# When a gated tile's copy may start, and who makes the last T sums

## What is computed

```python
x = attn_out.transpose(0, 2, 1, 3).reshape(B * S, H * D)   # 1536 x 512
for e in range(4):
    h = np.maximum(x @ w1[e], 0.0)
    out += p[:, e:e + 1] * (h @ w2[e])
h = out @ w_in
g = h * (1.0 / (1.0 + np.exp(-1.702 * h)))
return g @ w_out
```

## Time and profile before

| | |
|---|---|
| runs | 826.63, 828.28, 823.92 us (median 826.63) |
| profiled execution | 824.39 us, of which the span 822.2 us |
| TensorE clock granted | 0.998 of full speed over the span, 9 tenths or more in each of 40 slices |
| PE, DVE, ACT, POOL busy | 97%, 69%, 52%, 71% of the span |
| DMA | 148.92 MB, mean 181 GB/s |

### The profile page before, as it was taken

How to read it: one execution, slowest core, us unless ns; L and a number is a source line. 1 busy time by engine, 2 the same in 40 slices (tenths; PEclk the granted TensorE clock), 3 DMA queues, 4 the chain that set the end, 5 groups by cost and what they waited for, 6 DMA issues and landing times.

```text
span 822.2 us, 14168 instructions
## 1 busy us (share of the span) xinstructions
PE 798.7 (97%) x4894; PEld 779.6 (95%) x4894; DVE 568.6 (69%) x1194; ACT 427.8 (52%) x943; POOL 580.8 (71%) x406
## 2 busy tenths in 40 slices
PE   5889999999999999999999999999999999999997
PEld 4778999999999999999999999999999999999997
DVE  5888656666665566687877877665666665677777
ACT  3865445445445454546545544434456553656663
POOL 3697765655666699678778685777488873588794
PEclk9999999999999999999999999999999999999999
DMA  9959547375444354446245343343544445373412
GB/s 265 285 122 338 214 196 235 141 262 216 159 179 175 141 214 161 171 155 232 104 184 198 122 198 142 142 189 143 217 160 187 175 172 205 104 293 143 165 66 77
DMA packets 39957, 148.92 MB, mean 181 GB/s; under 512 B 16208, under 2 KB 17360, under 8 KB 36688
## 3 DMA queue, kind: packets, MB, share of 16 engines
q1 hardware_dynamic: 39888, 148.03, 49.9%
HBM read 100.81 MB, written 47.21 MB: 180 GB/s over the span
## 4 chain that ended last, share of the span: by engine, by line
PE 76%; POOL 10%; issue 5%; ACT 4%; DVE 3%; DMA 1%; SPq 0%; ACTq 0%; DVEq 0%; POOLq 0%
PE bank L1651 25%; PE bank L1653 24%; PE bank L1652 24%; POOL wd_lo L809 2%; POOL h_raw L832 2%; POOL t_raw L832 2%; PE bank L1606 2%; ACT prob L949 1%; PE bank L1617 1%; PE bank L1643 1%; DMA v_cols<-v_t 1%; ACT xb_first_hi L1050 1%; POOL wu_lo L730 1%; POOL wd_lo L742 1%; ACT xb_last_hi L1074 0%
## 5 line engine op out<-in xcount | busy, mean ns | idle before, releaser
L1358 DVE TENSOR_TENSOR xa<-bank,xa 128x384 f32<-128x384 f32 x208 | 115.8, 556 | 136.7 <-PE bank L1653 133.9
L1651 PE MATMUL bank<-h_hi,wd_hi 128*128 128x384 f32 x448 | 150.5, 336 | 0.3 <-DVE xa L1356 0.2
L1653 PE MATMUL bank<-h_lo,wd_hi 128*128 128x384 f32 x448 | 149.8, 334 | 0.0
L1652 PE MATMUL bank<-h_hi,wd_lo 128*128 128x384 f32 x448 | 149.7, 334 | 0.0
L1040 ACT ACTIVATE h_hi<-bank 128x384 fp32r<-128x384 f32 x112 | 55.1, 492 | 136.9 <-DVE bank L1415 113.5
L742 POOL TENSOR_TENSOR wd_lo<-stage,wd_hi 128x1024 fp32r<-128x1024 f32 x27 | 65.2, 2413 | 82.9 <-ACT wd_hi L997 82.8
L809 POOL TENSOR_TENSOR wd_lo<-stage,wd_hi 128x512 fp32r<-128x512 f32 x60 | 85.9, 1437 | 40.2 <-ACT wd_hi L1087 39.5
L1651 PE MATMUL bank<-xb_other_hi,wu_hi 128*128 128x384 f32 x336 | 113.0, 336 | 0.8 <-ACT snap L1024 0.2
L1653 PE MATMUL bank<-xb_other_lo,wu_hi 128*128 128x384 f32 x336 | 112.3, 334 | 0.0
L1652 PE MATMUL bank<-xb_other_hi,wu_lo 128*128 128x384 f32 x336 | 112.3, 334 | 0.0
L1024 ACT ACTIVATE snap<-bank 128x384 f32<-128x384 f32 x141 | 69.2, 491 | 64.0 <-PE bank L1653 63.1
(11 more groups left out here) (120 smaller groups left out, 2078.7 us busy)
## 6 DMA issues: line engine op xcount, KB each, us to landing
stage<-weights SPq DMA_DIRECT2D x25, 1024.0 KB, 4.9
split<-wu_hi SPq DMA_DIRECT2D x24, 896.0 KB, 3.6
split<-wu_lo SPq DMA_DIRECT2D x24, 896.0 KB, 5.6
wu_hi<-split SPq DMA_DIRECT2D x23, 896.0 KB, 6.3
wu_lo<-split SPq DMA_DIRECT2D x23, 896.0 KB, 8.0
stage<-weights SPq DMA_DIRECT2D x23, 512.0 KB, 4.5
k_win<-k_w SPq DMA_DIRECT2D x8, 720.0 KB, 8.1
v_win<-v_w SPq DMA_DIRECT2D x8, 576.0 KB, 9.3
```

The source lines that it names most:

```text
L1358: nc.vector.tensor_tensor(at, y_bank(g, t), at, ALU.add).then_inc(y_taken, 1)
L1651: nc.tensor.matmul(dst, w_h, a_h, start=first, stop=False, skip_group_check=True)
L1652: nc.tensor.matmul(dst, w_l, a_h, start=False, stop=False, skip_group_check=True)
L1653: return nc.tensor.matmul(dst, w_h, a_l, start=False, stop=last, skip_group_check=True)
```

## The change

It has two parts.

**Behind pairs.** In the first step of a pair, the raw copy of C11 and C21 (column 0 of row 0) waits for T sum 1 of the pair before (`4 * q - 3`) and no longer for all four and for the low tiles. In the second step, C11 and C21 wait for the low part of T sum 4 alone, C22 and C12 for T sum 3. Also, in the last layer (g >= 32), DVE takes P2,0 before the low part of C12 and no longer behind it.

**The tail.** T sums 2 and 3 of the last pair are made by DVE, in two halves each, straight from the gated tile's bank (`sum_last`), and the raw copies of C22 and C12 of step 47 go. POOL makes T sum 4 and its low part. The takes of the last pair have an order of their own, `TAKES_LAST`: P1,1 goes far back, P6,0 ahead of P3,1, and P2 behind P7. PE's order stays.

```diff
+TAKES_LAST = (("P1", 0), ("P5", 0), ("P5", 1), ("P1", 1), ("P3", 0), ("P6", 0), ("P3", 1), ("P6", 1),
+              ("P7", 0), ("P7", 1), ("P2", 0), ("P2", 1), ("P4", 0), ("P4", 1))
...
         def taken(g0, name, d):
 
-            return takes(g0) + TAKES.index((name, d)) + 1
+            return takes(g0) + (TAKES_LAST if g0 == STEPS - 2 else TAKES).index((name, d)) + 1
...
-                    pool.wait_ge(tsum_done, at + 2)
+                    if g + 2 == STEPS:
+                        pool.wait_ge(tlast_done, 3)
+                        pool.wait_ge(raw_done, copied(g + 1, "C21"))
+                    else:
+                        pool.wait_ge(tsum_done, at + 2)
...
-            for n in (2, 3, 4):
-                sum_hidden(STEPS - 2, n)
+
+            sum_hidden(STEPS - 2, 4)
+            pool.wait_ge(thi_done, 4 * pair_of(STEPS - 2) + 4)
+            pool.wait_ge(tlo_done, 4 * pair_of(STEPS - 2) + 3)
+            hi, lo = moved_2(5)
+            nc.gpsimd.tensor_tensor(lo, hidden_sum(4), hi.bitcast(F32), ALU.subtract).then_inc(tlo_done, 1)
...
                 act.wait_ge(gated_done, ready(g, c))
+                if g + 1 == STEPS and c[2] == "2":
+
+                    act.wait_ge(tlast_done, {"C22": 2, "C12": 3}[c])
...
-                if c[2] == "1":
-                    wait_count(act, blo_done if g % 2 == 0 else tlo_done, len(TILES_2) * q if g % 2 == 0 else 4 * q)
-                    wait_count(act, tsum_done, 4 * q)
+                if c[2] == "1" and g % 2 == 0:
+                    wait_count(act, tsum_done, 4 * q - 3)
                 elif g % 2 == 0:
                     wait_count(act, tlo_done, 4 * q - 1)
-                else:
-                    wait_count(act, tsum_done, 4 * q)
+                elif c[2] == "1":
+                    wait_count(act, tlo_done, 4 * q)
+                else:
+                    wait_count(act, tsum_done, 4 * q - 1)
...
-                act.wait_ge(tsum_done, 4 * pair_of(g) + n)
+                if g + 2 == STEPS and n in (2, 3):
+                    act.wait_ge(tlast_done, n + 1)
+                elif g + 2 == STEPS and n == 4:
+                    act.wait_ge(tsum_done, 4 * pair_of(g) + 2)
+                else:
+                    act.wait_ge(tsum_done, 4 * pair_of(g) + n)
...
-                    copy_tile(g, "C22")
+                    if g + 1 < STEPS:
+                        copy_tile(g, "C22")
...
-                    copy_tile(g, "C12")
+                    if g + 1 < STEPS:
+                        copy_tile(g, "C12")
...
+            def sum_last(n, c):
+
+                f = int(c[1]) - 1
+                dve.wait_ge(gated_done, ready(STEPS - 1, c))
+                b = hidden_sum(1) if n == 2 else hidden_block(0, 1)
+                nc.vector.tensor_tensor(hidden_sum(n)[:, f, :], hidden(STEPS - 1, c), b[:, f, :], ALU.subtract
+                                        ).then_inc(tlast_done, 1)
...
                     take_product(g - 2, "P5", 1)
-                    low_tile(g - 1, "C12")
+                    if g < FFN0:
+                        low_tile(g - 1, "C12")
                     take_product(g - 2, "P2", 0)
+                    if g >= FFN0:
+                        low_tile(g - 1, "C12")
```

More of the change, by code:

```diff
@@ L262, in attention_moe_ffn @@
         tlo_done = sem("tlo_done")
+        tlast_done = sem("tlast_done")
         y_done = sem("y_done")
@@ L366, in takes, with summed @@
             return sum((len(TAKES) - IN_PAIR if x % 2 else IN_PAIR) if paired(x) else 8 for x in range(g))
+        def summed(g0, name, d):
+            return takes(g0) + TAKES.index((name, d)) + 1
         def taken(g0, name, d):
-            return takes(g0) + TAKES.index((name, d)) + 1
+            return takes(g0) + (TAKES_LAST if g0 == STEPS - 2 else TAKES).index((name, d)) + 1
         def plain(g):
@@ L417, in copied @@
         def copied(g, c):
+            if g + 1 == STEPS:
+                return 4 * (2 * pair_of(g) + 1) + {"C11": 1, "C21": 2}[c]
             return 4 * (2 * pair_of(g) + g % 2) + READY[c]
@@ L672, in _ @@
                         sp.dma_start(out[d, :, 0:SEQ], xa[0][:, d, :]).then_inc(out_done, 16)
-            for name, d in TAKES[IN_PAIR:]:
-                if name != "P3":
+            for name, d in TAKES_LAST:
+                if name in ("P2", "P6", "P7", "P4"):
                     i, c, first = ADDED[name]
@@ L1045, in high_tile @@
                 act.wait_ge(gated_done, ready(g, c))
+                if g + 1 == STEPS and c[2] == "2":
+                    act.wait_ge(tlast_done, {"C22": 2, "C12": 3}[c])
                 if paired(g0 - 1):
-                    act.wait_ge(y_done, taken(g0 - 2, {(0, "1"): "P1", (1, "1"): "P2", (1, "2"): "P3"}[g % 2, c[2]], 1))
+                    act.wait_ge(y_done, summed(g0 - 2, {(0, "1"): "P1", (1, "1"): "P2", (1, "2"): "P3"}[g % 2, c[2]], 1))
                 else:
@@ L1067, in high_sum @@
             def high_sum(g, n):
-                act.wait_ge(tsum_done, 4 * pair_of(g) + n)
+                if g + 2 == STEPS and n in (2, 3):
[4 more added lines that the diff above has]
+                    act.wait_ge(tsum_done, 4 * pair_of(g) + n)
                 if paired(g - 1):
-                    act.wait_ge(y_done, taken(g - 2, ("P5", "P6", "P7", "P4")[n - 1], 1))
+                    act.wait_ge(y_done, summed(g - 2, ("P5", "P6", "P7", "P4")[n - 1], 1))
                 else:
@@ L1083, in high_held @@
                 if paired(g - 1):
-                    act.wait_ge(y_done, taken(g - 2, name, 1))
+                    act.wait_ge(y_done, summed(g - 2, name, 1))
                 else:
@@ L1360, in take_product @@
             def take_product(g, name, d):
-                dve.wait_ge(y_done, taken(g, name, d))
+                dve.wait_ge(y_done, summed(g, name, d))
                 if name == "P6":
@@ L1495, in _ @@
                     gate(g, "C22")
[L1496 to L1502, removed]
-                        take_product(g - 1, "P5", 0)
+                    if g + 1 < STEPS:
+                        take_product(g - 1, "P5", 0)
+                        gate(g, "C21")
+                        add_c12(g)
+                        low_tile(g, "C21")
+                        gate(g, "C12")
+                        low_tile(g, "C22")
                     continue
@@ L1573, in _ @@
                     key_maxima(u)
+            sum_last(3, "C22")
+            gate(STEPS - 1, "C21")
+            add_c12(STEPS - 1)
+            sum_last(2, "C22")
+            low_tile(STEPS - 1, "C21")
+            gate(STEPS - 1, "C12")
+            sum_last(2, "C12")
+            take_product(STEPS - 2, "P5", 0)
+            low_tile(STEPS - 1, "C22")
+            low_tile(STEPS - 1, "C12")
             take_product(STEPS - 2, "P5", 1)
-            low_tile(STEPS - 1, "C12")
-            take_product(STEPS - 2, "P2", 0)
-            take_product(STEPS - 2, "P2", 1)
+            sum_last(3, "C12")
             low_sum(STEPS - 2, 2)
-            take_product(STEPS - 2, "P3", 0)
-            take_product(STEPS - 2, "P3", 1)
+            take_product(STEPS - 2, "P1", 1)
             low_sum(STEPS - 2, 3)
[L1582 to L1585, removed]
+            for name, d in TAKES_LAST[4:]:
                 take_product(STEPS - 2, name, d)
```

## The result

| | before | changed |
|---|---|---|
| median of 20 runs | 824.96 us (823.30 to 829.14) | 820.60 us (818.61 to 825.24) |
| ratio | | 0.9946, 95% interval 0.9935 to 0.9957 |
| span of the profiled execution | 822.2 us | 818.8 us |
| granted clock, mean | 0.998 | 0.992 |

The kernel is 4.5 us faster (0.54%; the interval is 3.5 to 5.4 us). Forecast were 5.9 us and a time of 820.7. The time hit, the gain is 1.4 us smaller; the median of the three runs that the forecast was taken from, 826.63, was 1.7 above that of 20 runs, which hid the miss.

The account below looks back on a forecast made before the run. PE, busy for 97% of the span, was taken as the bound, with gains only at its stops: 3.2 + 1.0 + 1.7 = 5.9 us off a 826.63 us median, forecast 820.7 (own range 818.5 to 822.5; eight in ten 817.0 to 824.3).

Parts of the forecast that it names:

- What bounds the kernel: Whole kernel: PE is busy 97% of the span, so gains come only where PE stands still or does less.
- Part one: Behind expert pairs: C11's earlier copy removes the stops at P7 and P7,0, 5 x 0.65 = 3.2 us.
- the room that I gave P7,0: Expert pairs: P3,1 and P6,0 taken by 391.5, where P7,0 wants that at 392.55; 1.0 us of room.
- Part two: Last layer, steps 42, 44, 46: P2,0 taken ahead of C12's low part removes P2,1's stop, 1.0 us.
- The list of what would be wrong: Signs: PE still waiting at P7, tail two-tile low part over 1.5 us, new stop at P3,0 or next pair's P1,0.
- Part three: Tail: P3,0 0.3 us late, P6,0 and P7,0 without waits, P4,1 1.8 earlier; 1.7 us in all.
- The rule on the shared port: Tail: two-SBUF-input DVE and SBUF-reading POOL instructions block each other; sums from banks cost 0.56 us whatever POOL does.
- A: Rival, tail: DVE's low parts meet POOL or a take sits between; 821.7 to 822.4 us, chance 0.12.
- B: Rival, expert pairs: one stop stays, 822.3 us; both stay, 823.9 us; chance 0.12.
- C: Rival: removed waits weren't the last ones and the tail's new sums cost their saving; 826.6 us, chance 0.03.
- D: Rival, tail: sums from banks as slow as 1.94 us, kernel slower, 829.4 us if part one gives nothing; chance 0.03.
- faster: Whole kernel: a gain past about 0.5%, here 4.1 us, that a measurement can tell from no change; chance 0.74.

Follow-up runs that it names:

- e1: Kernel before with only the new waits of the raw copies (`copy_tile`): ratio 0.9954 (0.9935 to 0.9972).
- e2: Kernel before with only P2,0 taken ahead of C12's low part in the last layer: ratio 0.9994 (0.9979 to 1.001).
- e4: Changed kernel without taking P2,0 ahead of C12's low part in the last layer: ratio to before 0.9933 (0.9908 to 0.9958).
- e9: Changed kernel with one more DVE instruction behind the tail's first sum: 0.47 us more up to P4,1.
- e10: Kernel before with `keep(g, 1)` ahead of C11's raw copy behind the expert pairs: steps 16 to 28 take 176.06 us, before 175.98.
- e5: Changed kernel with P4,0 taken ahead of C12's gate in the last layer: step 40 to the tail's P2,0 115.57 us, changed kernel 116.36.
- e3: Kernel before with only the tail's part of the change: ratio 0.9985 (0.9967 to 1.0003).
- e6: Changed kernel, POOL's weight sums of pairs 42, 44, 46 on 8 of 256 columns, rest left out: step 40 to P2,0 115.33 us, changed kernel 116.36.
- e7: Like e5, with `keep(g, 1)` ahead of P6's weights on ACT in step 47: ratio to before 0.9918 (0.9893 to 0.9943).
- e11: Like e7, with T sum 3's halves behind C22's and C12's low parts, P3,0's take ahead of T sum 3's low part: ratio to before 0.9925.

## Why the prediction was right, and where not

**What bounds the kernel.** Right: PE's stops were the whole of it, and every gain is one of them gone. Not right is that each stop is worth its length: that at P2,1 was worth nothing.

**Part one.** Right in place, path and size. Predicted were `keep` done 0.5 us before PE wants it (it is 0.6) and 3.2 us in all (3.16 in the changed kernel, 3.25 alone). One link came out better than I had it: T sum 3's low part, taken at 1.94 us as in the earlier trace rows, took 0.95, because it now begins 0.06 us before POOL's next sum and not into it (389.19 and 389.25 above); POOL's sum took 2.04 instead of 1.28. It is so in all five of these steps (0.95, and 2.02 to 2.04). So the room that I gave P7,0 was too small by a microsecond.

**Part two.** The step that failed is the term "0.26 us of stall and about 0.07 of slow start go, three times: 1.0 us". The mechanism at P2,1 was right (its step is 1.04 now), but I asked only what is due directly behind the swap (C11's adding, P5), and not what is late one step on. The low part of T sum 4 was in the trace before, at 1.16 us, beside a weight sum of POOL (761.02, above); P4,0's take ended 0.15 us before P1,0 of the pair began, and where PE waited for a take 0.14 to 0.15 passed from its end to the product's start (750.59 to 750.73, 764.39 to 764.54): no room at all. The list of what would be wrong named a stop "at P1,0 of the next pair", but no chance or term stood behind it. The measured term is 0.0, and e1, e2 and e4 show it from both sides; what came in its place is the new stop at P1,0, 0.25 and 0.29 us, and that at P7 of step 47, 0.21.

**Part three.** 1.67 us from P2,0 to P4,1, against 1.8 forecast (0.3 lost ahead of P3,0 and 2.1 gained from there; measured from there, 9.54 - 7.63 = 1.9). P6,0 and P7,0 have lost their waits, the sums from banks take 0.56 us, the low parts of T sums 2 and 3 0.94. The loss is there, nearly 0.3 in all as forecast, but only 0.16 of it is at P3,0; 0.05 and 0.07 are at P2,0 and P2,1, which I had taken for on time. That room was as narrow as P1,0's, and e9 shows that it was none.

**The rule on the shared port**, which I weighed in part three from the Trainium skill ("SBUF — State Buffer", Who interferes with whom), held wherever the traces show it: the sum from a bank at 801.95 has 0.56 us, although POOL works until 802.97, and two-tile instructions block each other (numbers in the last section). I had used it where the change adds instructions and not where it shifts them against POOL, and there it decided part two.

**The rivals.** None of A to D came. What came is a case that I hadn't listed, the wait that takes the place of the one removed, though that is the first one to look for.

**The numbers.** 820.6 lies in the range, 818.5 to 822.5, but that it met 820.7 to 0.1 us is luck: a start 1.7 us too high and a gain 1.4 us too large cancelled. The gain of 0.54% is just over the bound of 0.5% for "faster", which had 0.74, and its interval, 0.43 to 0.65%, takes in that bound.

## What to carry to other kernels

When PE is 97% busy and a stop of 0.3 us is removed, look for the chains on other engines that didn't wait at that stop: they stay where they are, and the next place where PE meets them has that much less room. Compare the room there (here: when the take ends against when the product is due, 0.0 us) before counting the gain. A stop is worth removing at the instruction that all later ones hang on; e10 and e2 took away the first of a row and got nothing, e1 and e5 took away the link.

## What the hardware showed

- A low part with two tiles (0.95 us alone) that DVE begins while POOL sums tiles doesn't show as idle: it shows as a longer instruction, up to 2.14 us, whose end is tied to that of POOL's. Of the 40 low parts of T sums in the trace of the kernel before, 32 end 0.81 or 0.82 us behind a POOL instruction, wherever they began; 6 began less than 0.1 us before POOL's end and took 0.95; 2 met none. If DVE begins 0.06 us first, it takes 0.95 and POOL's sum of 1.28 takes 2.04. So the order of the two starts decides who pays: 1.0 us on DVE (1.94 against 0.95) or 0.75 on POOL.
- The end of the span, from P4,1's start, is 4.1 to 4.2 us in the traces of before, changed, e1, e3, e4, e5, e9 and e10, and 5.2 to 5.3 in those of e2, e6, e7 and e11. The tail of e2 is that of before. In these four traces a 16 KB transfer on the queue that the profile calls "q8 instruction" falls into the last outputs: it begins between 0.4 us before P4,1's start and 0.8 us behind it and takes 1.5 to 1.8 us. The other eight have none there (in e4 one ends 1.1 us before P4,1). In e6, e7 and e11 SP issues the third last output 0.8 to 1.0 us later than in the changed kernel; in e2 all are issued on time and the data lands 1.0 us later. Whether that transfer is the cause isn't tested.
- The stretch up to step 16 varied by 3.8 us between the twelve traces used, whose instructions there are the same (323.05 to 326.87), with the clock granted between 0.75 and 0.91 from 40 to 50 us. That is nearly as much as the whole change gives; only the comparison stretch by stretch made 0.1 us readable.
